# Linear attention, gated feed-forward and four attention experts on one core: scores of head pairs without the later quarter, block-diagonal values, k loaded by halves, and the experts' mask over 128 rows

## Chip, cores and metric

One core of one Trainium2 chip runs the whole program. The metric is the device time of one execution in microseconds; less is better. The kernel before has a median of 767.92 us over three runs (767.56 to 768.51).

## What is computed

Four batches (B = 4) of 768 tokens pass through three stages, all in float32.

1. Linear attention of 8 heads with head size 48. With a complex decay a, brought to a magnitude of at most 0.999, a state of 48 x 48 per head follows `S_t = a_t * S_(t-1) + k_t v_t^T`, and `y_t = q_t . Re(S_t)`.
2. Feed-forward: `h = relu(x @ w_in)` of width 1024, a convolution over 3 tokens, a sigmoid of it as a gate, and `(h * gate) @ w_out`, which has width 384.
3. Four experts of one attention head each (size 64) with a causal mask. Scores are `q k^T / 8`, softmax over keys, `@ v @ wo`; each token adds the two experts with the highest gate logits, weighted.

## The kernel before, in words

**Chunks.** The recurrence is worked out in 6 chunks of 128 tokens (NC, CH). The cumulative products of the decays are taken from the middle of a chunk outwards, so q and k are scaled once and inside a chunk the outputs are a masked product: scores = k^T q (L1427), multiplied by a 0/1 mask (L1086) and used as the moving operand of a product with v. A token of a chunk lies in one of two halves of 64 (HALF), so that partitions 0 to 63 of a chunk's tokens are its first half and 64 to 127 its second. What came before the chunk enters through a state `st` of 96 rows (real and imaginary part of 48).

**One chunk on TensorE** (`main` of the tensor block): `scores(c+1)`, 8 products of 96 rows x 128 keys x 128 queries into two PSUM banks; `transpose_k(c+1)`, 8 transposes (L1414); `rotate(c)` (L1451); `outputs(c, 0)`; `gain(c+1)`, 8 products of 128 tokens x 96 x 48 columns (L1439); `outputs(c, 1)`; `outputs(c, 2)`. An output block packs four products with 32 stationary columns side by side into the array (L1478 with v as stationary operand, L1476 with the state). Blocks 0 and 1 take the first or last 32 columns of v of four heads each, block 2 the remaining 16 of each head in pairs that are summed, over columns padded with zeros. Every f32 product that is no transpose is two instructions in the trace.

**One chunk on the other engines.** VectorE masks the scores in two instructions, one per four heads (`mask`, L1086), and makes the state of the next chunk (L1104, L1119, L1122, L1124) and the low part of x (`x_low`, L1095). ScalarE copies the transposed k (`copy_k`, L639) and the outputs (`copy_x`, L647). In batches 1 and 2 it does parts of the next batch's decays between chunks: after `copy_x` of chunk 3 it loads a table, takes square roots (L596), loads another table, takes a logarithm and an exponential (L600, L605), and only then comes to `copy_x` of chunk 4.

**Queues.** All transfers are issued by SyncE (SP), in program order. q and k are stored scaled to DRAM, and `load_heads(b, c)` fetches a chunk of them by head into one of three slots (L496), as four transfers of 48 rows: q and k, real and imaginary. A slot is free when the outputs of the chunk three before are ready. In batch 0 the stores of units 1 and 2 (`store_first_chunk`, `store_unit`, L483, L473) and the loads of the next batch's decays (`load_a`, L439) stand between the loads of the chunks.

**Experts.** Twelve steps t per batch, each with two query tiles (sides 0 and 1) that together see 7 x 128 keys. `expert_scores(t)` makes the scores of side 1, adds the mask to them (`later`, L1591), then makes those of side 0 (512 keys at most per product, so two products where it has 768 or 640 keys) and masks these. An expert's q and k lie in 64 rows of the array, and the experts of the two sides always lie in different halves. The mask is a product of two bf16 operands of 64 rows, in two instructions. The order of the work is written out by hand: in step t, TensorE makes the scores of t + 2, transposes the probabilities of t (L1617), and makes a product with v every second time (L1633) and the output projection (L1641).

The functions that the change touches:

## Time and profile before

| | |
|---|---|
| median of the runs | 767.92 us (767.56 to 768.51) |
| the profiled execution | 768.12 us |
| its span in the profile | 766.2 us |
| TensorE busy with products | 671.0 us, 88% of the span |
| TensorE busy with weight loads (beside the products) | 511.4 us, 67% |
| VectorE busy | 614.7 us, 80% |
| ScalarE busy | 409.2 us, 53% |
| chain that ended last, by engine | TensorE 45%, VectorE 36%, ScalarE 8%, DMA 5% |

The profile lists busy time per engine. A product's duration contains its way through the array, so products overlap in it, and what a product costs in a stream is read from the distance of the starts or from the chain of waits. That chain is followed back from the last instruction: each piece was released by the end of the one before it. A batch takes 168 us in the steady state: linear attention about 41 us, the feed-forward stage 54 us and 23 us with the projections, the experts 50 us. "PE" is TensorE, "PEld" its weight loads, "DVE" VectorE, "ACT" ScalarE, "SPq" the queue of SyncE.

### The profile page before, as it was taken

Reading aid. Unit: us, or ns where it says so; the run is one execution under the profiler, and the core shown is the slowest. Engines: PE = TensorE matmul, PEld = TensorE weight load, DVE = VectorE, ACT = ScalarE, POOL = GpSimd, SP = SyncE. Lnnn points to the kernel's source line nnn. Section 1 sums busy time; section 2 is a strip of 40 time slices with the busy share of each in tenths; the row PEclk is TensorE's granted clock in tenths of the full one; section 3 lists DMA queues with packets and bytes.
Section 4 is the critical chain, followed back from the end, with each engine's and each line's share of the span. In section 5 each row is a group of like instructions: output and inputs, shape, how many; then the busy total and the mean of one; then the engine's idle time right before and its main releaser. Section 6 shows DMA issues by size and latency. Waiting matters only on the chain.

```text
span 766.2 us, 13280 instructions
## 1 busy us (share of the span) xinstructions
PE 671.0 (88%) x5274; PEld 511.4 (67%) x5274; DVE 614.7 (80%) x1165; ACT 409.2 (53%) x747; POOL 0.2 (0%) x4
## 2 busy tenths in 40 slices
PE   0006868799999999999999999999999999999998
PEld 0003657676656778876656788876667788998765
DVE  3999876899889878899888878899888675773563
ACT  6304237633757854533757756434766434664565
POOL 0000000000000000000000000000000000000000
PEclk9999898999999999999999999999999999999999
DMA  8604684310018473500028653300027440000001
GB/s 345 254 0 119 175 234 138 123 42 0 1 41 227 148 197 75 178 29 1 0 63 248 175 158 111 139 1 0 1 86 224 126 121 8 1 1 1 1 22 42
DMA packets 93629, 73.85 MB, mean 96 GB/s; under 512 B 8704, under 2 KB 85760, under 8 KB 92928
## 3 DMA queue, kind: packets, MB, share of 16 engines
q1 hardware_dynamic: 93568, 73.01, 31.4%
q8 instruction: 42, 0.69, 0.4%
q14 instruction: 19, 0.16, 0.1%
HBM read 49.34 MB, written 23.65 MB: 95 GB/s over the span
## 4 chain that ended last, share of the span: by engine, by line
PE 45%; DVE 36%; ACT 8%; DMA 5%; issue 3%; SPq 2%; DVEq 0%; ACTq 0%
DVE cv L1131 7%; PE wide L1582 5%; PE wide L1563 5%; PE bank L1633 4%; PE bank L1641 4%; PE wide L1617 4%; PE wide L1427 4%; DVE m L949 3%; DVE heads L1136 3%; PE wide L1439 3%; DMA heads_dram<-araw 3%; DVE m L948 2%; DVE nmax L1195 2%; PE wide L1558 2%; DVE W L961 2%
## 5 line engine op out<-in xcount | busy, mean ns | idle before, releaser
L1492 PE MATMUL wide<-x_hi_lo,win_hi 128*128 128x384 f32 x384 | 108.9, 353 | 7.9 <-DVE x_hi_lo L1095 6.6
L1492 PEld LDWEIGHTS wide<-x_hi_lo,win_hi 128*128 128x128 f32 x384 | 70.7, 190 | 12.5 <-issue 8.5
L1513 PE MATMUL wide<-heads,wout 128*128 128x384 f32 x200 | 70.7, 496 | 4.1 <-DVE heads L1136 4.0
L1195 DVE TENSOR_REDUCE nmax<-wide 128x1 f32<-128x768 f32 (+2 forms) x96 | 55.3, 618 | 23.3 <-PE wide L1591 23.1
L1131 DVE SCALAR_TENSOR_TENSOR cv<-h,wconv,cv 128x768 f32<-128x768 f32 x64 | 64.9, 1014 | 8.2 <-ACT cv L679 6.7
L1582 PE MATMUL wide<-attn 64*128 64x512 f32 (+3 forms) x256 | 65.0, 482 | 2.3 <-ACT attn L703 2.3
L727 ACT ACTIVATE xs<-wide 128x896 f32<-128x896 f32 x48 | 44.1, 919 | 41.6 <-PE wide L1617 41.6
L1492 PE MATMUL wide<-x_hi_lo,win_lo 128*128 128x384 f32 x192 | 65.1, 339 | 0.0
L1427 PE MATMUL wide<-heads 96*128 96x128 f32 x384 | 52.0, 292 | 10.3 <-DMA heads<-heads_dram 10.3
L684 ACT ACTIVATE cv<-cv 128x768 f32<-128x768 f32 x32 | 27.1, 845 | 58.3 <-DVE cv L1131 58.1
L1427 PEld LDWEIGHTS wide<-heads 96*128 96x128 f32 x384 | 48.3, 203 | 14.8 <-DMA heads<-heads_dram 11.0
L1401 PE MATMUL wide<-attn,ident 128*128 128x512 f32 x4 | 3.1, 860 | 62.2 <-ACT m L621 62.2
L1513 PEld LDWEIGHTS wide<-heads,wout 128*128 128x128 f32 x200 | 36.2, 189 | 30.9 <-DVE heads L1136 11.0
L657 ACT ACTIVATE h<-wide 128x384 f32<-128x384 f32 x64 | 29.0, 489 | 50.7 <-DVE heads L1136 39.2
L1633 PE MATMUL bank<-xs,attn 128*64 128x128 f32 x672 | 46.4, 279 | 0.2 <-ACT xs L727 0.2
L1086 DVE TENSOR_TENSOR attn<-wide,cmask 128x512 f32<-128x512 f32 x48 | 31.3, 682 | 17.2 <-PE wide L1427 17.2
L1633 PEld LDWEIGHTS bank<-xs,attn 128*64 128x64 f32 x672 | 35.8, 136 | 13.5 <-ACT xs L727 8.1
L1401 PEld LDWEIGHTS wide<-attn,ident 128*128 128x128 f32 x4 | 1.0, 289 | 63.0 <-issue 63.0
L1582 PEld LDWEIGHTS wide<-attn 64*128 64x128 f32 x256 | 25.5, 184 | 24.1 <-issue 9.9
L718 ACT ACTIVATE cv<-wide,nmax 128x768 f32<-128x768 f32 (+2 forms) x48 | 37.9, 790 | 1.0 <-DVE nmax L1195 0.5
L1617 PE MATMUL wide<-ident,cv 128*128 128x128 f32 x240 | 36.6, 283 | 2.0 <-DVE cv L1210 2.0
L1492 PEld LDWEIGHTS wide<-x_hi_lo,win_lo 128*128 128x128 f32 x192 | 36.6, 190 | 2.0
(205 smaller groups left out, 1512.6 us busy)
## 6 DMA issues: line engine op xcount, KB each, us to landing
heads<-heads_dram SPq DMA_DIRECT2D x96, 192.0 KB, 3.5
araw<-a_in SPq DMA_DIRECT2D x12, 768.0 KB, 6.2
araw<-qk_in SPq DMA_DIRECT2D x12, 768.0 KB, 4.8
heads_dram<-m SPq DMA_DIRECT2D x18, 384.0 KB, 3.4
heads_dram<-araw SPq DMA_DIRECT2D x18, 384.0 KB, 4.0
v<-v_in SPq DMA_DIRECT2D x4, 1536.0 KB, 6.6
out_dram<-h SPq DMA_DIRECT2D x24, 192.0 KB, 2.5
heads_dram<-m SPq DMA_DIRECT2D x12, 192.0 KB, 3.5
```

What stands on the lines that cost most here:

```text
L718: nc.scalar.activation(prob[side][:, t % 2, 0:n], slot_scores(t, side), ACT.Exp, bias=nmax[:, t, side:side + 1], accum_out=zsum[:, t, side ...
L727: nc.scalar.activation(probT[:, t % PROBT, :], wide[2][:, 0:KEYS], ACT.Copy).then_inc(s_pc, 1)
L1086: TT(sc[:, c % 2, 4 * quad:4 * quad + 4, :], low[2 + quad].rearrange("p (h t) -> p h t", h=4), cmask[:].unsqueeze(1).broadcast_to([P, 4, P ...
L1131: STT(cb, hb[:, tap:tap + S], wconv[:, mt, tap:tap + 1], cb, ALU.mult, ALU.add).then_inc(s_c, 1)
L1195: dve.tensor_reduce(nmax[:, t, side:side + 1], slot_scores(t, side), AXX, ALU.max, negate=True).then_inc(s_nm, 1)
L1427: last = MM(low[2 + quad][:, hh * P:(hh + 1) * P], k_of(c, hd), q_of(c, hd), start=True, stop=True)
L1492: last = MM(low[u % 2][:, 0:NT], w[:, k, mt * P:(mt + 1) * P], xs[:, k, n * NT:(n + 1) * NT], start=(k == 0 and part == 0), stop=(k == KT ...
L1513: last = MM(mlp_bank[u][:, 0:NT], wout[:, mt, k * P:(k + 1) * P], hgate(mt)[:, n * NT:(n + 1) * NT], start=(mt == 0), stop=(mt == MT - 1))
L1563: last = MM(bank_u[:, 0:NT], w[:, k, i * P:(i + 1) * P], xT[:, k, n * NT:(n + 1) * NT], start=(k == 0), stop=(k == KT - 1))
L1582: MM(slot_scores(t, side)[:, lo:hi], qT[rows, e // 2, i * P:(i + 1) * P], kT[rows, e // 2, lo:hi], start=True, stop=hi != keys(t, side))
L1617: last = nc.tensor.transpose(dst[:, j * P:(j + 1) * P], prob[side][:, t % 2, j * P:(j + 1) * P], ident[:])
L1633: last = MM(out_bank[side][rows, o:o + P], vx[:, j, e * HD:(e + 1) * HD], probT[:, (t + r) % PROBT, span(t, side)][:, j * P:(j + 1) * P], ...
```

## The change

- **Scores.** A pair of heads gets three squares of a half chunk each instead of two full 128 x 128 squares: in one PSUM strip of 192 columns the rows 0 to 63 belong to the first head of the pair and 64 to 127 to the second. Keys of the first half meet all 128 queries, keys of the second half only the 64 later queries. There are 16 products with 64 stationary columns where 8 had 128.
- **Mask.** VectorE multiplies the two outer planes of each strip in one instruction (512 columns, mask in bf16); ScalarE copies the middle plane (`copy_scores`, 256 columns), which needs no mask. TensorE's next scores and outputs wait for this copy (semaphore s_sf), and the copy waits for the mask. In ScalarE's order `copy_scores(b, 0)` comes first in a batch, and `copy_scores(b, c+1)` after `copy_k(b, c+1)`.
- **Values.** v is stored block-diagonally: for each pair and half, 128 rows (two heads x 64 tokens) by 96 columns, 4608 columns per partition in place of 3072. `gain` has 8 products of 96 columns where 8 had 48. Output blocks 0 and 1 take 64 stationary columns of a pair and half, with 128 or 64 query columns; block 2 takes the last 32 columns of each pair. The state's products in blocks 0 and 1 become 6 per block in place of 4, in block 2 4 in place of 8. The weights w_in are reordered to match.
- **k by halves.** `load_heads` issues six transfers in place of four: k comes in two halves of 64 tokens.
- **Experts' mask.** `later` is one product over all 128 rows in place of two over 64, and for side 1 it now comes after the first product of side 0. The wait for it before the second product of side 0 stays.
- Small things: lf, gt, the gates' small buffers and the third staging buffer of w_in lie in other buffers; the mask constants are fewer; `keep_busy` has 384 columns in place of 512; the mask is cast to bf16 once, before the first `mask`.

The core of the diff:

```diff
@@ -81,6 +81,8 @@
 SHORT = PAIRS * P
 KEYS = (NC + 1) * P
 PROBT = 4
+PAIR = 3 * HALF
+HEAD_PARTS = 16 * 6
 HOLD = 3
...
@@ -103,11 +105,10 @@
         ident = sb("ident", [P, P])
-        negated = sb("negated", [P, P])
-        cmask = sb("cmask", [P, P])
+        cmask = sb("cmask", [P, P], BF16)
         rot = sb("rot", [2 * D, 2 * D])
         tie = sb("tie", [P, E * E])
...
@@ -288,6 +289,7 @@
         s_te = sem("k_tokens_copied")
         s_s = sem("scores_ready")
         s_se = sem("scores_masked")
+        s_sf = sem("scores_copied")
...
@@ -348,8 +350,13 @@
         def groups(part):
             return part.rearrange("p (n i g) -> p n i g", i=GROUP, g=GROUP)
-        def k_of(c, hd):
-            return qk_slot[:, c % SLOTS_A, 1, hd, :]
+        def k_half(c, half):
+            return qk_slot[:, c % SLOTS_A, 1, half * H // 2:(half + 1) * H // 2, :].rearrange("d h t -> d (h t)")
+        def k_of(c, hd, half):
+            return k_half(c, half)[:, hd * HALF:(hd + 1) * HALF]
...
@@ -359,6 +366,23 @@
             return t[:, hd, 0:D]
+        def pair_values(c, p, half):
+            return v[:, c, p, half, :]
+        def pair_scores(p):
+            return wide[1][:, p * 2 * P:p * 2 * P + PAIR]
+        def pair_planes(t, size):
+            return t.rearrange("p (n x) -> p n x", x=size)[:, :, 0:PAIR].rearrange("p n (r x) -> p n r x", x=HALF)
...
@@ -491,10 +515,14 @@
                     sp.wait_ge(s_sto[c // UNIT_CHUNKS], 64 * (b + 1))
                 if c >= SLOTS_A:
                     sp.wait_ge(s_y, NC * b + c - SLOTS_A + 1)
-                for x in range(2):
-                    for part in range(2):
-                        sp.dma_start(qk_slot[part * D:(part + 1) * D, c % SLOTS_A, x, :, :],
-                                     qk_dram[x, part, c].rearrange("(h d) t -> d h t", d=D)).then_inc(s_hd[c % SLOTS_A], 16)
+                for part in range(2):
+                    rows = slice(part * D, (part + 1) * D)
+                    sp.dma_start(qk_slot[rows, c % SLOTS_A, 0, :, :],
+                                 qk_dram[0, part, c].rearrange("(h d) t -> d h t", d=D)).then_inc(s_hd[c % SLOTS_A], 16)
+                    for half in range(2):
+                        sp.dma_start(k_half(c, half)[rows].rearrange("d (h t) -> d h t", h=H),
+                                     qk_dram[1, part, c, :, half * HALF:(half + 1) * HALF]
...
@@ -639,6 +667,15 @@
                     nc.scalar.activation(ktok[:, c % 2, part * DM:(part + 1) * DM], low[part][:, 0:DM],
                                          ACT.Copy).then_inc(s_te, 1)
+            def copy_scores(b, c):
+                act.wait_ge(s_se, NC * b + c + 1)
+                if c >= 2:
+                    act.wait_ge(s_y, NC * b + c - 1)
+                nc.scalar.activation(pair_planes(sc[:, c % 2].rearrange("p h t -> p (h t)"), PAIR)[:, :, 1, :],
+                                     pair_planes(wide[1][:], 2 * P)[:, :, 1, :], ACT.Copy).then_inc(s_sf, 1)
             def copy_x(b, c):
...
@@ -742,9 +779,13 @@
             def main(b):
                 more = b + 1 < B
+                if b:
+                    copy_scores(b, 0)
                 for c in range(NC):
                     if c + 1 < GAINS:
                         copy_k(b, c + 1)
+                    if c + 1 < NC:
+                        copy_scores(b, c + 1)
                     if b and more and c < UNITS - 1:
...
@@ -888,6 +929,7 @@
             w_squares(0, 2)
             w_ln(0, 2)
             w_guess(0, 2)
+            copy_scores(0, 0)
             for b in range(B):
...
@@ -1078,14 +1120,15 @@
                     TT(araw[:, x, cols], araw[:, x, cols], w_re[:, cols], ALU.mult).then_inc(done, 1)
             def mask(b, c):
-                for quad in range(2):
-                    n = 2 * (NC * b + c) + quad
-                    dve.wait_ge(s_s, n + 1)
-                    if c >= 2:
-                        dve.wait_ge(s_y, NC * b + c - 1)
-                    TT(sc[:, c % 2, 4 * quad:4 * quad + 4, :],
-                       low[2 + quad].rearrange("p (h t) -> p h t", h=4),
-                       cmask[:].unsqueeze(1).broadcast_to([P, 4, P]), ALU.mult).then_inc(s_se, 1)
+                dve.wait_ge(s_s, NC * b + c + 1)
+                if c >= 2:
+                    dve.wait_ge(s_y, NC * b + c - 1)
+                TT(pair_planes(sc[:, c % 2].rearrange("p h t -> p (h t)"), PAIR)[:, :, 0::2, :],
+                   pair_planes(wide[1][:], 2 * P)[:, :, 0::2, :],
+                   cmask[:].rearrange("p (r x) -> p r x", x=HALF).unsqueeze(1).broadcast_to([P, H // 2, 2, HALF]),
+                   ALU.mult).then_inc(s_se, 1)
...
@@ -1375,6 +1417,9 @@
                 products_by_chunk(u, 0)
                 if u == 1:
                     w_sumsq(0, UNITS - 1)
+                    dve.wait_ge(s_const, 64)
+                    dve.tensor_copy(cmask[:], staged[:, 0:P]).then_inc(s_cast, 1)
+                    dve.wait_ge(s_cast, 3)
                     mask(0, 0)
...
@@ -1391,7 +1436,7 @@
                 for _ in range(n):
-                    MM(b6[:], ident[:], mask_parts, start=True, stop=True)
+                    MM(b6[:, 0:3 * P], ident[:], staged, start=True, stop=True)
...
@@ -1407,26 +1452,30 @@
                 n = 2 * (GAINS * b + c) + part
                 if part == 0:
-                    pe.wait_ge(s_hd[c % SLOTS_A], 64 * (2 * b + c // SLOTS_A + 1))
+                    pe.wait_ge(s_hd[c % SLOTS_A], HEAD_PARTS * (2 * b + c // SLOTS_A + 1))
                 if c:
                     pe.wait_ge(s_te, n - 1)
-                for hh in range(4):
-                    last = nc.tensor.transpose(low[part][:, hh * 2 * D:(hh + 1) * 2 * D], k_of(c, 4 * part + hh),
-                                               ident[0:2 * D, 0:2 * D])
+                for i in range(4):
+                    p, half = 2 * part + i // 2, i % 2
+                    last = nc.tensor.transpose(low[part][:, i * 2 * D:(i + 1) * 2 * D],
+                                               k_half(c, half)[:, p * P:(p + 1) * P], ident[0:2 * D, 0:2 * D])
                 last.then_inc(s_t, 1)
             def scores(b, c):
-                for quad in range(2):
-                    n = 2 * (NC * b + c) + quad
-                    if c and quad == 0:
-                        pe.wait_ge(s_hd[c % SLOTS_A], 64 * (2 * b + c // SLOTS_A + 1))
-                    if c:
-                        pe.wait_ge(s_se, n - 1)
-                    for hh in range(4):
-                        hd = 4 * quad + hh
-                        last = MM(low[2 + quad][:, hh * P:(hh + 1) * P], k_of(c, hd), q_of(c, hd),
-                                  start=True, stop=True)
-                    last.then_inc(s_s, 1)
+                if c:
+                    pe.wait_ge(s_hd[c % SLOTS_A], HEAD_PARTS * (2 * b + c // SLOTS_A + 1))
+                    pe.wait_ge(s_sf, NC * b + c)
+                for p in range(H // 2):
+                    for half in range(2):
+                        for r in range(2):
+                            hd = 2 * p + r
+                            cols = slice(P * half, P * half + (HALF if half else P))
+                            last = MM(pair_scores(p)[r * HALF:(r + 1) * HALF, cols],
+                                      k_of(c, hd, half), q_of(c, hd)[:, half * HALF:],
+                                      start=True, stop=True)
+                last.then_inc(s_s, 1)
             def gain(b, c):
@@ -1435,9 +1484,11 @@
                 else:
                     pe.wait_ge(s_u, GAINS * b + c)
                 pe.wait_ge(s_te, 2 * (GAINS * b + c) + 2)
-                for hd in range(H):
-                    last = MM(b5[0:2 * D, hd * D:(hd + 1) * D], ktok[:, c % 2, hd * 2 * D:(hd + 1) * 2 * D],
-                              values(v[:, c], hd), start=True, stop=True)
+                for p in range(H // 2):
+                    for half in range(2):
+                        i = 2 * p + half
+                        last = MM(b5[0:2 * D, p * 2 * D:(p + 1) * 2 * D], ktok[:, c % 2, i * 2 * D:(i + 1) * 2 * D],
+                                  pair_values(c, p, half), start=half == 0, stop=half == 1)
                 last.then_inc(s_z, 1)
             def rotate(b, c):
@@ -1462,20 +1513,36 @@
                         pe.wait_ge(s_fe[0], PAIRS * b + 1)
                     if c:
                         pe.wait_ge(s_st, GAINS * b + c)
-                if block < 2:
-                    pe.wait_ge(s_se, 2 * n + block + 1)
-                take = remaining if block == 2 else leading
-                heads_of = [[4 * block + g for g in range(4)]] if block < 2 else [[2 * g + r for g in range(4)] for r in range(2)]
+                if block == 0:
+                    pe.wait_ge(s_sf, n + 1)
                 o = y_bank[c % 2][:, block * P:(block + 1) * P]
-                for part in range(2 if c else 1):
-                    for r, some in enumerate(heads_of):
-                        first_one, last_one = part == r == 0, (part == 1 or c == 0) and r == len(heads_of) - 1
-                        for g, hd in enumerate(some):
-                            dst = o[g * LEAD:(g + 1) * LEAD, :]
-                            if part:
-                                last = MM(dst, take(st[:, c % 2], hd), q_of(c, hd), start=first_one, stop=last_one)
-                            else:
-                                last = MM(dst, take(v[:, c], hd), sc[:, c % 2, hd, :], start=first_one, stop=last_one)
+                for g in range(2 if block < 2 else 4):
+                    p = 2 * block + g if block < 2 else g
+                    rows, cols = ((slice(2 * LEAD * g, 2 * LEAD * (g + 1)), slice(0, 2 * LEAD)) if block < 2 else
+                                  (slice(LEAD * g, LEAD * (g + 1)), slice(2 * LEAD, 3 * LEAD)))
+                    first_half, second_half = (pair_values(c, p, half)[:, cols] for half in range(2))
+                    some = sc[:, c % 2, p, :]
+                    if c:
+                        MM(o[rows, :], first_half, some[:, 0:P], start=True, stop=False)
+                    else:
+                        MM(o[rows, 0:HALF], first_half, some[:, 0:HALF], start=True, stop=True)
+                        MM(o[rows, HALF:P], first_half, some[:, HALF:P], start=True, stop=False)
+                    last = MM(o[rows, HALF:P], second_half, some[:, P:PAIR], start=False, stop=c == 0)
+                if c:
+                    state = st[:, c % 2]
+                    if block < 2:
+                        pairs = (2 * block, 2 * block + 1)
+                        parts = ([(2 * g, leading(state, 2 * p), 2 * p, True) for g, p in enumerate(pairs)]
+                                 + [(2 * g + 1, remaining(state, 2 * p + r), 2 * p + r, r == 1)
+                                    for r in range(2) for g, p in enumerate(pairs)])
+                    else:
+                        parts = [(p, leading(state, 2 * p + 1), 2 * p + 1, True) for p in range(H // 2)]
+                    for g, weights, hd, ends in parts:
+                        last = MM(o[g * LEAD:(g + 1) * LEAD, :], weights, q_of(c, hd), start=False, stop=ends)
                 if block == KT - 1:
                     last.then_inc(s_y, 1)
...
@@ -1585,17 +1652,14 @@
                 def later(side):
-                    i, e = query_tile(t, side), expert(t, side)
-                    rows = slice(HD * (e % 2), HD * (e % 2) + HD)
-                    for r in range(2):
-                        last = MM(slot_scores(t, side)[:, i * P:(i + 1) * P], mask_h[rows, r * P:(r + 1) * P],
-                                  mask_h[rows, (2 + r) * P:(3 + r) * P], start=False, stop=r == 1)
-                    return last
+                    i = query_tile(t, side)
+                    return MM(slot_scores(t, side)[:, i * P:(i + 1) * P], mask_h[:, 0:P], mask_h[:, P:2 * P],
+                              start=False, stop=True)
                 n = keys(t, 0)
                 products(1, 0, keys(t, 1))
+                products(0, 0, 512)
                 later(1).then_inc(s_sh, 1)
-                products(0, 0, 512)
                 if n > 512:
                     pe.wait_ge(s_sh, SLOTS * b + t + 1)
```

## Rows read from the trace of the kernel before

**Rows 1.** Busy time by stage: us, then PE, PEld, DVE, ACT, POOL busy, clock, DMA share, GB/s.
```profile
433.00:474.00 41.00, 40.71 (x613) 34.33 (x611) 33.32 (x58) 23.76 (x38) 0.00 (x0) 1.00 0.49 131
614.60:621.41 6.81, 6.81 (x108) 5.79 (x107) 5.02 (x9) 2.39 (x5) 0.00 (x0) 1.00 0.44 116
```

**Rows 2.** Chain of waits, one chunk of batch 3: start us, us, what.
```profile
614.60 1.98 PE wide L1427 x16
616.58 0.66 PE wide L1414 x8
617.24 0.65 PE bank L1451 x2
617.89 0.36 PE bank L1478 x8
618.25 0.22 PE bank L1476 x8
618.47 1.49 PE wide L1439 x16
...
620.53 0.44 PE bank L1478 x16
620.97 0.44 PE bank L1476 x16
```

**Rows 3.** The same chain in batch 1: scores at its start, a wait in its second chunk.
```profile
265.24 1.81 PE wide L1427 x16
...
280.11 5.85 DMA heads<-heads_dram
```

**Rows 4.** Timeline of the SP queue in batch 0: start us, us, operation, transfers.
```profile
77.91 1.86 SPq L496 DMA_DIRECT2D heads<-heads_dram  x4
...
80.87 1.32 SPq L483 DMA_DIRECT2D heads_dram<-araw  x2
...
116.57 2.10 SPq L496 DMA_DIRECT2D heads<-heads_dram  x4
118.78 0.55 SPq L439 DMA_DIRECT2D araw<-a_in  x1
```

**Rows 5.** Timeline of ScalarE in batches 0 and 2; in brackets its idle time.
```profile
125.17 1.49 ACT L591 ACTIVATE m<-araw 128x1536 f32<-128x1536 f32 x1 [0.38 <-DMA araw<-a_in]
...
441.24 0.49 ACT L741 ACTIVATE h<-bank 128x384 f32<-128x384 f32 x1 [0.80 <-PE bank L1641]
...
468.33 1.28 ACT L596 ACT_TABLE_LOAD   x1
...
473.50 0.86 ACT L647 ACTIVATE x_hi_lo<-wide 128x192 fp32r<-128x192 f32 x2
```

**Rows 6.** Timeline of TensorE in batch 2: start of the second chunk's scores, end of the stage.
```profile
441.04 1.95 PE L1427 MATMUL wide<-heads 96*128 96x128 f32 x16
...
472.17 0.43 PE L1478 MATMUL bank<-attn,v 128*32 128x128 f32 x8 [0.29 <-issue]
...
476.41 0.41 PE L1492 MATMUL wide<-x_hi_lo,win_hi 128*128 128x384 f32 x1 [0.51 <-DVE x_hi_lo L1095]
```

**Rows 7.** Timeline of TensorE, one step of the experts in batch 3.
```profile
730.79 0.71 PE L1582 MATMUL wide<-attn 64*128 64x256 f32 x3
731.33 0.22 PE L1591 MATMUL wide<-mask_h 64*128 64x128 bf16 x1
...
731.77 0.38 PE L1582 MATMUL wide<-attn 64*128 64x128 f32 x2
...
732.19 0.76 PE L1617 MATMUL wide<-ident,cv 128*128 128x128 f32 x5
```

**Rows 8.** Groups by form: copies and masks; count, busy us, mean ns, idle before.
```profile
L697 ACT ACTIVATE attn<-wide 128x256 f32<-128x256 f32 x16 | 6.1, 384 | 5.1 <-PE wide L1558 3.7 <-PE wide L1554 1.3
L1086 DVE TENSOR_TENSOR attn<-wide,cmask 128x512 f32<-128x512 f32 x48 | 31.3, 682 | 17.2 <-PE wide L1427 17.2
```

**Rows 9.** The page's transfers: KB each, median us from issue to landing.
```profile
heads<-heads_dram SPq DMA_DIRECT2D x96, 192.0 KB, 3.5
```

86 lines of the change are left out of this document (41 added, 45 removed).

## The prediction

> **What bounds the kernel now.** I read the stages first, then the chain of waits, then the timelines at the places where the change puts something new. In the linear attention of a steady batch the stage table has TensorE busy for 40.71 of 41 us, VectorE for 33.32, ScalarE for 23.76; in one chunk of 6.81 us TensorE has no gap at all [rows 1]. The chain says the same: all ten pieces of a chunk are products (the two left out repeat the 0.36 and 0.22), and they add up to those 6.81 us [rows 2]. So in this stage a microsecond counts if it is TensorE's; the vector engine's 5.02 us per chunk lie beside it. Three places differ. In batch 0 the chain runs through SP's queue and its transfers, up to the load of decays at 118.78 that releases ScalarE at 125.17 [rows 4, 5]. In batch 1 it waits once 5.85 us for a chunk's heads [rows 3]. At the end of batches 1 and 2 it runs through ScalarE, which after chunk 3's copy does 5.2 us of the next batch's decays before it copies chunk 4 [rows 5]. In the experts' later steps it is TensorE again.
>
> **What a product costs here.** A chunk's scores take 16 instructions in 1.81 us where no changeover of the array precedes them, 0.111 to 0.113 us each with 128 stationary and 128 moving columns [rows 3]; after packed products they take 1.98, so a changeover costs about 0.15. The gain has 96 stationary and only 48 moving columns, and its 16 still take 1.49 us, less the changeover 0.084 each: 0.87 ns per stationary column, so there the weights set the pace, and scores are at the same 0.87 ns per column [rows 2]. Packed products with 32 stationary and 128 moving columns come every 0.0275 us, a quarter of 0.11 [rows 2]. I take the rule that an instruction costs the larger of 0.85 ns per stationary column and 0.85 ns per moving column over the number of products side by side.
>
> **The change, TensorE's part.** Scores: 32 instructions of 64 stationary columns, 0.054 each by that rule, 1.73 us against 1.78: -0.05. The quarter that is left out shortens only the moving side; if weights of neighbouring tiles load at the same time, the price is (16 x 0.054 + 16 x 0.027) = 1.3 us, -0.5. Nearest row is the gain, weight-bound, so I take -0.05. The transposes after the scores now follow a packed product: one changeover, +0.12 (0 to 0.2, from the 0.17 between the two score rows). Output blocks 0 and 1: the values' 8 instructions have 64 stationary columns, 0.43 against 0.22, +0.21 each (+0.1 if moving columns count); the state's products with 32 columns follow those with 64, +0.12 each if this is a changeover (0 to 0.17), and are 12 in place of 8, +0.11 each (+0.2 if the two that share 32 columns of the array queue up). Block 2: the values stay at 16 instructions, 0.44 by the weights; the state's halve, -0.22. The gain keeps 96 stationary columns and gets 96 moving ones: 0 by the rule; the transposes with 128 stationary and 96 moving columns run at 0.66/8 = 0.083, which also fits [rows 2]; +0.1 at worst. Sum: -0.05 + 0.12 + 0.42 + 0.24 + 0.22 - 0.22 = +0.7 us per chunk (-0.3 to +1.3). Chunk 0 has no state, but its first product is split in two, so that blocks have 12, 12 and 24 instructions in place of 8, 8 and 16: about +0.9 with scores and changeover.
>
> At the changeover between tile widths the rows show 1.98 against 1.81 us for the same scores [rows 2, 3], but no row has 64 columns followed by 32. The Trainium skill, TensorEngine Tiling (Array Packing), section Key Properties, says that changing the tiling mode, not merely the tile, drains the engine; by it both widths in a block cost as in my sum. Without it the sum would be 0.24 less per chunk. The same section says that different tiles can load weights and multiply in parallel, which speaks for the lower price of the scores; that is a rival below.
>
> On the path lie, in batches 1 to 3, three chunks 0 (2.7 us), nine full chunks (two in batch 1, three in batch 2, four in batch 3; 6.3 us) and the outputs of batch 3's last chunk (0.6): **+9.6**. Batch 0's chunks lie under its transfers, and the chunks 4 and 5 of batches 1 and 2 under ScalarE's chain, counted next.
>
> **The new waits on ScalarE.** (a) Start of a batch: scores of chunk 1 now wait for the copy of chunk 0's middle plane, which stands behind the last output copy of the batch before. That copy runs from 441.24 to 441.73 [rows 5]; 256 columns take 0.384 [rows 8]; with the hand-over the scores start at about 442.2 in place of 441.04 [rows 6]: +1.2, three times, **+3.6**. The mask is done long before, and behind the waiting TensorE stands only its own order. (b) End of batches 1 and 2: the copy for chunk 5 stands behind the decays of the next batch, that is from 473.5 [rows 5]. Chunk 5's outputs started at 472.17 [rows 6]; now they start at 473.5 + 0.45 + 0.05 = 474.0 plus what the chunks before are late. They take 2.6 us, copy and low part 0.9 each, so the first product that needs chunk 5 starts at 478.6 in place of 476.41 [rows 6]: 2.2, and the table load behind the copy adds 0.2: +2.4, twice, **+4.8**. (c) In the other chunks the copy has a whole chunk's time; hidden by TensorE's 6.8 us, and 0.4 us per chunk if that cover were gone.
>
> **SP's queue.** An issue takes 1.86 / 4 to 2.10 / 4 us, 0.5 [rows 4]. Two more per chunk: in batch 0 the loads of chunks 0 and 1 push the four stores behind them from the end of the load at 79.8 to 81.9; two of these had waited for VectorE until 80.87 and now start at 82.9, +2.0. Chunks 2 to 5 add 1.0 each, all ahead of the load at 118.78, and ScalarE had only 0.38 us idle there [rows 4, 5]. **+6.0**. ScalarE must also have copied chunk 5's plane before these squares; that is about as late, 0 to +2, taken in the range. In batch 1 the wait of 5.85 us [rows 3] begins 1.0 later and its transfers have half the row length for k: **+1.2**. Elsewhere a chunk's load takes 0.35 + 5 x 0.5 + 3.5 to 5.85 us (median landing [rows 9], and this row), 6.4 to 8.7, against a period of 7.5; at the median it fits.
>
> **The experts.** In a step with 640 keys TensorE needs 1.40 us from the first scores to the transposes [rows 7]. Side 1's scores and side 0's run beside each other in different halves of rows, so side 0 sets the time: about 0.1 + 0.85 + 0.21 + mask. Now the mask over 128 rows waits until both have drained (0.1), passes through (0.22 [rows 7]), and only its end releases the next product (weights and hand-over 0.13), then the array changes over twice (0.2) and one mask instruction instead of two is saved (0.06): 1.8 us, +0.4, the same with 768 keys; without a second product (512 keys) about 0. Eight steps of batch 3 are bound by TensorE: 3.2. In batches 0 to 2 the first two are (0.8), four more are bound by VectorE and TensorE alike (half, 0.8), the others hidden: 4.8. **+8.0** (0 to 13).
>
> **Costed at nothing:** 24 masks fewer on VectorE, 0.68 us each [rows 8], hidden under TensorE, and worth 0.65 once before the first chunk, against the cast of the mask; v's larger rows and the moved small buffers lie in front of loads that the feed-forward stage covers; 384 columns in `keep_busy` fill a wait for a transfer. If the cover of v's load were gone it would cost its extra 0.8 MB, some 3 us per batch at the rate of its own loads.
>
> Sum: 9.6 + 3.6 + 4.8 + 6.0 + 1.2 + 8.0 = 33.2 on the profiled 768.12 us: 801.3. The median of the runs is 0.2 lower, so **801 us**.
>
> **Rivals.**
> - *The tiles load side by side and changing width is free.* Then scores fall by 0.5, values' blocks rise by 0.2 together and block 2 falls by 0.1: with the one changeover -0.3 per chunk in place of +0.7, chunk 0 at 0. For it: 32-column products at 0.0275 would also come out so. Against it: the gain. Nothing outside the loop changes: 33.2 - 12.8 = 20.4, **788**. Chance 0.27.
> - *The heads' transfers become the bound.* If they land in 5.85 us as in batch 1 [rows 3], a chunk takes 8.7 us in place of 7.5, three chunks in each of three batches: +10, **811**. Against it: the median landing of 3.5 [rows 9]. Chance 0.12.
> - *VectorE was the real pace of the loop.* Freed of one mask per chunk, 0.64 x 18 = 11.5 us less, **757**, if none of the additions shows. It decides once a chunk's masks, not its products, end last; at 5.02 of 6.81 us busy, and with no VectorE piece in the chain [rows 1, 2], little speaks for it. Chance 0.06.
> - *Gains and waits cancel*, 768, which needs the weights' rule and the queue's both wrong. Chance 0.03.
> - My forecast: 0.52.
>
> **Numbers.** The range reaches from below the first rival (experts' step at nothing: 780) to above the second with batch 0's extra wait (817). Within 0.2%, 1.5 us, is what a measurement of this kernel can't tell from no change. Faster 0.06, same 0.03, slower 0.91.
>
> **What would show it.** The score group: 768 instructions with 64 stationary columns at 0.05 us apart, or at 0.04. The chunk period in batch 3: 7.5 us, against 6.5 for the first rival. A ScalarE wait of 1.2 us before the scores of chunk 1, and chunk 5's outputs released by ScalarE's copy in batches 1 and 2. The start of the products with w_in in batch 0 some 6 us later. An idle 0.3 to 0.5 us behind the mask product in each expert step with 640 or 768 keys. If the period is below 6.8 or the time below 780, the price per stationary column was wrong.

## The result and the profile after

The changed kernel has a median of 803.01 us over four runs (802.2 to 805.07), the kernel before in the same series 768.08. The ratio is 1.0454, with a 95% interval of 1.0431 to 1.0476: slower, 2.0 us above the forecast of 801.0 and inside the range. The profiled execution has a span of 800.9 us, 34.7 more than before; the comparisons by stage below are made with spans. One execution of experiment 4 and one of experiment 5 lie far above the others of their kernel; their medians are those of the other three, and both are named below.

The page of the changed kernel: span, busy time per engine, chain by engine, the group of the row maxima (count, busy us, mean ns, idle before and its releaser), and the heads' transfers.

```profile
span 800.9 us, 14033 instructions
PE 701.2 (88%) x5626; PEld 511.3 (64%) x5626; DVE 602.2 (75%) x1142; ACT 416.2 (52%) x771; POOL 0.2 (0%) x4
PE 51%; DVE 28%; ACT 8%; DMA 6%; issue 4%; SPq 3%; DVEq 0%; ACTq 0%
L1238 DVE TENSOR_REDUCE nmax<-wide 128x1 f32<-128x768 f32 (+2 forms) x96 | 55.3, 618 | 33.6 <-PE wide L1656 33.5
heads<-heads_dram SPq DMA_DIRECT2D x48, 192.0 KB, 3.0
heads<-heads_dram SPq DMA_DIRECT2D x96, 96.0 KB, 3.2
```

TensorE is busy 30 us longer and its share of the chain rises from 45% to 51%, while VectorE's busy time falls by 12.5 us and its share of the chain from 36% to 28%. The time still rose: the loop had no VectorE piece in its chain before [rows 2], so the masks that VectorE was spared could give little back there. Transfers of k with half the rows' length and half the bytes land in 3.2 us, against 3.5 for whole ones before [rows 9]: they did not become the bound.

**One chunk in batch 3**, in the chain of waits (start us, us, what). It answers to [rows 2].

```profile
644.24 1.49 PE wide L1475 x32
645.73 0.81 PE wide L1460 x8
646.54 0.65 PE bank L1502 x2
647.18 0.38 PE bank L1528 x4
647.56 0.11 PE bank L1532 x4
647.67 0.57 PE bank L1545 x12
648.25 1.53 PE wide L1490 x16
649.78 0.38 PE bank L1528 x4
650.15 0.11 PE bank L1532 x4
650.27 0.36 PE bank L1545 x8
...
651.43 1.09 PE wide L1475 x21
```

The period is 651.43 - 644.24 = 7.19 us against 6.81. Piece by piece: scores 1.49 against 1.98 (-0.49), transposes 0.81 against 0.66 (+0.15), values of block 0 0.49 against 0.36 (+0.13), its state 0.57 against 0.22 (+0.35), gain +0.04, blocks 1 and 2 together 1.65 against 1.45 (+0.20). The sum is +0.38; TensorE still has no gap.

**The three stages of each batch.** From the timelines of TensorE I took the first score, the first product with w_in, the first projection, and the next batch's first score. (Of batch 0 the first two stages stand together.) The feed-forward stage has the same length in both within 0.1 us. The column "more" is taken before rounding. Each row comes from one profile, and moves a little from profile to profile: experiments 5, 6, 7 and 9 below change nothing in batch 0 up to the projections (7 only an order inside the chunk), and there it takes 200.7, 200.4, 203.8 and 202.6 us.

| stage | before | after | more | forecast |
|---|---|---|---|---|
| batch 0 up to the projections | 197.1 | 202.1 | +5.0 | +6.0 |
| attention, batch 1 | 41.3 | 45.8 | +4.5 | +7.1 |
| attention, batch 2 | 40.6 | 46.7 | +6.1 | +6.6 |
| attention, batch 3 | 40.5 | 44.2 | +3.6 | +5.5 |
| projections and experts, batch 0 | 68.0 | 74.4 | +6.4 | +1.6 |
| batch 1 | 68.0 | 72.1 | +4.1 | +1.6 |
| batch 2 | 68.0 | 70.4 | +2.4 | +1.6 |
| batch 3, to the end | 70.7 | 73.6 | +2.9 | +3.2 |

The rows add to 35.0, with the rounding of the feed-forward stages 34.7. The forecast total was near, its parts were not: attention cost 5 us less than it said, the experts 8 more, nearly all in batches 0 and 1. There the chain of the changed kernel has pieces that the kernel before does not have; this is batch 0's end:

```profile
256.95 4.03 DMA heads_dram<-araw
261.00 0.33 SPq L520
...
263.94 6.10 DMA araw<-a_in
...
271.45 0.91 ACT xs L764
```

VectorE's products for the next batch end later, their store lands later, SP then issues six loads of heads (2.9 us), and behind them the second third of the decays of batch 2 at 263.94, and ScalarE's squares wait for that. In the kernel before, the same load was issued 10.1 us sooner, of which batch 0's late start explains 5.0:

```profile
253.84 0.55 SPq L439 DMA_DIRECT2D araw<-a_in  x1
```

The transposed probabilities (L764) stand behind the squares. ScalarE's timeline has the wait in brackets:

```profile
270.06 1.48 ACT L619 ACTIVATE m<-araw 128x1536 f32<-128x1536 f32 x1 [2.28 <-DMA araw<-a_in]
```

### The profile page after: what moved, and what is told of

Its sections match the earlier page's. It is cut to its first block, busy times and chain, and to the rows that moved or that the text cites. A ratio compares the mean times of both kernels' runs of the same rounds, so it can differ in the third digit from the quotient of the medians.

```text
span 800.9 us, 14033 instructions
## 1 busy us (share of the span) xinstructions
PE 701.2 (88%) x5626; PEld 511.3 (64%) x5626; DVE 602.2 (75%) x1142; ACT 416.2 (52%) x771; POOL 0.2 (0%) x4
## 4 chain that ended last, share of the span: by engine, by line
PE 51%; DVE 28%; ACT 8%; DMA 6%; issue 4%; SPq 3%; DVEq 0%; ACTq 0%
PE wide L1649 8%; DVE cv L1174 7%; PE wide L1630 4%; PE bank L1697 4%; PE wide L1681 4%; DMA heads_dram<-araw 3%; PE wide L1475 3%; DVE m L991 3%; PE wide L1490 3%; PE bank L1705 3%; DVE heads L1179 3%; PE wide L1559 2%; DVE m L990 2%; DMA araw<-a_in 2%; PE wide L1625 2%
## 5 line engine op out<-in xcount | busy, mean ns | idle before, releaser
L1238 DVE TENSOR_REDUCE nmax<-wide 128x1 f32<-128x768 f32 (+2 forms) x96 | 55.3, 618 | 33.6 <-PE wide L1656 33.5
L1649 PE MATMUL wide<-attn 64*128 64x512 f32 (+3 forms) x256 | 73.1, 495 | 4.2 <-ACT attn L740 2.3
L1580 PE MATMUL wide<-heads,wout 128*128 128x384 f32 x200 | 70.7, 496 | 4.2 <-DVE heads L1179 4.2
L764 ACT ACTIVATE xs<-wide 128x896 f32<-128x896 f32 x48 | 44.0, 917 | 49.5 <-PE wide L1681 49.5
L1475 PE MATMUL wide<-heads 96*64 96x128 f32 (+1 forms) x768 | 39.9, 260 | 10.9 <-DMA heads<-heads_dram 8.0
L1475 PEld LDWEIGHTS wide<-heads 96*64 96x64 f32 x768 | 36.7, 144 | 16.5 <-DMA heads<-heads_dram 8.5
L1681 PE MATMUL wide<-ident,cv 128*128 128x128 f32 x240 | 34.9, 276 | 4.0 <-ACT xs L764 4.0
L1580 PE MATMUL bank<-heads,wout 128*128 128x384 f32 x100 | 36.3, 486 | 0.0
```

What stands on the lines that cost most here:

```text
L764: nc.scalar.activation(probT[:, t % PROBT, :], wide[2][:, 0:KEYS], ACT.Copy).then_inc(s_pc, 1)
L1238: dve.tensor_reduce(nmax[:, t, side:side + 1], slot_scores(t, side), AXX, ALU.max, negate=True).then_inc(s_nm, 1)
L1475: last = MM(pair_scores(p)[r * HALF:(r + 1) * HALF, cols], k_of(c, hd, half), q_of(c, hd)[:, half * HALF:], start=True, stop=True)
L1580: last = MM(mlp_bank[u][:, 0:NT], wout[:, mt, k * P:(k + 1) * P], hgate(mt)[:, n * NT:(n + 1) * NT], start=(mt == 0), stop=(mt == MT - 1))
L1649: MM(slot_scores(t, side)[:, lo:hi], qT[rows, e // 2, i * P:(i + 1) * P], kT[rows, e // 2, lo:hi], start=True, stop=hi != keys(t, side))
L1681: last = nc.tensor.transpose(dst[:, j * P:(j + 1) * P], prob[side][:, t % 2, j * P:(j + 1) * P], ident[:])
```

## The experiments

Twelve kernels ran. "Before" was run beside each set of four: median 769.27 us beside experiments 1 to 4, 768.66 beside 5 to 8 and 768.95 beside 9 to 12. No kernel leaves computation out.

**1. k by halves alone**, on the kernel before (wait counts adapted):

```diff
-                for x in range(2):
-                    for part in range(2):
-                        sp.dma_start(qk_slot[... x, :, :], qk_dram[x, part, c] ...)
+                for part in range(2):
+                    sp.dma_start(qk_slot[rows, c % SLOTS_A, 0, :, :], qk_dram[0, part, c] ...)
+                    for half in range(2):
+                        sp.dma_start(qk_slot[rows, c % SLOTS_A, 1, :, cols], qk_dram[1, part, c, :, cols] ...)
```

> The kernel before, with each chunk's k loaded by halves of its tokens (six transfers of heads per chunk in place of four, rows of 256 bytes for k), everything else as before. Theory: SP's queue is on the path. In batch 0 ten of the added issues at 0.5 us stand ahead of the load of decays that ScalarE waits for, +5 us; in batch 1 the wait for chunk 3's heads grows by 1.2; and in the experts of batches 0 and 1 the decays' loads, which stand behind the heads' in the queue, may now be late for ScalarE, +0 to 4. So 774 to 778, and the start of the w_in products of batch 0 some 5 us later. Rival: the queue is late only together with TensorE's own delay; then 768 to 770.

Measured: 774.34 us (seven executions, 771.0 to 782.1), ratio 1.0082 (1.0039 to 1.0125). The size is right, the place is right only in part. Batch 0 up to the projections stays at 197.1: the load of decays that [rows 4] has at 118.78 is issued at 119.45, because SP's added issues filled time in which it had waited for stores. The cost came at the experts' end in batches 0 and 1 (70.2 and 72.8 in place of 68.0, 7.0 us in the profile, where 0 to 4 had been expected) and 1.0 in the attention of batches 1 and 2. The chain at the end of batch 1 has the pieces that were shown above for the changed kernel:

```profile
420.56 4.85 DMA heads_dram<-araw
...
429.05 5.98 DMA araw<-a_in
```

**2. The experts' mask alone**, on the kernel before: one product over 128 rows, for side 1 after the first product of side 0 (the mask's constants and the width of `keep_busy` follow).

```diff
-                    for r in range(2):
-                        last = MM(..., mask_h[rows, r * P:(r + 1) * P], mask_h[rows, (2 + r) * P:(3 + r) * P], ...)
+                    return MM(..., mask_h[:, 0:P], mask_h[:, P:2 * P], start=False, stop=True)
...
-                later(1).then_inc(s_sh, 1)
                 products(0, 0, 512)
+                later(1).then_inc(s_sh, 1)
```

> The kernel before with only the experts' mask of the change: one product over 128 rows, and for side 1 behind the first product of side 0. Theory: in steps with 640 and 768 keys the second product of side 0 waits for the mask to pass through the array; about +0.3 to 0.4 us in the steps that TensorE bounds, in all +6 to +10, 774 to 778, with a step of 640 keys in batch 3 at 1.8 us from scores to transposes in place of 1.40. Rival: the saved mask instructions pay for the wait; 766 to 769.

Measured: 779.5 us, ratio 1.0135 (1.0107 to 1.0162), 1.5 above the expected 774 to 778. The experts take 70.3, 71.5, 70.3 in batches 0 to 2 and 73.6 in batch 3: +2.3 to 2.9 where only the mask acts, and in batch 1 1.2 more by the load of decays (7.35 us in the chain).

**3. The same mask at its old place**, ahead of side 0's product:

> As the last one, but with the mask of side 1 in its old place, before the products of side 0. If the wait for the mask was the cost, this takes it away (it is covered by side 0's first product) and the time comes back to 766 to 770. If the cost is that a product over all 128 rows can't run beside the other side's, side 1 and side 0 now run one after the other: +0.3 to 0.7 us per step, in all 48 steps, so slower than the late order, 780 to 790.

Measured: 797.82 us, ratio 1.0375 (1.0336 to 1.0414), worse than any bound that I had set. The experts take 75.5 in batches 0 to 2, +7.5 each, and 78.9 to the end in batch 3, +8.2. TensorE's timeline of a step with 640 keys:

```profile
761.10 0.70 PE L1582 MATMUL wide<-attn 64*128 64x256 f32 x2
761.73 0.23 PE L1589 MATMUL wide<-mask_h 128*128 128x128 bf16 x1
761.89 1.34 PE L1582 MATMUL wide<-attn 64*128 64x512 f32 x4
...
763.24 0.72 PE L1614 MATMUL wide<-ident,cv 128*128 128x128 f32 x5
```

From the first score to the transposes it takes 2.14 us (before: 1.40 [rows 7]). The mask over 128 rows starts behind side 1's scores, and side 0's only start behind the mask, 0.79 us after side 1's: the two sides no longer run beside each other in their halves of the rows. At its late place the same mask cost 18 us less (experiment 2).

**4. The middle plane copied by VectorE**, on the changed kernel (ScalarE's calls of `copy_scores` taken out):

```diff
+                dve.tensor_copy(pair_planes(sc[...], PAIR)[:, :, 1, :],
+                                pair_planes(wide[1][:], 2 * P)[:, :, 1, :]).then_inc(s_sf, 1)
```

> The changed kernel with the middle plane of the scores copied by VectorE right behind its mask instruction; ScalarE has no part in it. Theory: the waits on ScalarE go: 0.9 us at the start of batches 1 to 3, and at the end of batches 1 and 2 about 3 us each with the slow clock behind it; in all -9 to -11, so 792 to 794, although VectorE has 0.4 us more per chunk. Rival: VectorE's added copy is on the path itself, or what is behind ScalarE's (its own decays) is as late; 799 to 803.

Measured: 790.0 us (three executions, 789.6 to 791.4), ratio 1.0277 (1.0244 to 1.0311), 13 us less than the changed kernel and below the 792 to 794 expected. A fourth execution, the profiled one, took 2368 us (see the end), so this kernel has no trace from which its stages can be read; experiments 8 and 10 contain the same edit.

**5. The first third of the decays ahead of the heads**, on the changed kernel:

```diff
+                    if b + 2 < B:
+                        load_a(b + 2, 0)
                     sp.wait_ge(s_p, len(PROJECTIONS) * (b + 1))
                     load_heads(b + 1, 0)
                     load_heads(b + 1, 1)
-                    if b + 2 < B:
-                        load_a(b + 2, 0)
```

> The changed kernel, but the load of the decays for the batch after next (its first third) is issued ahead of the twelve loads of heads of chunks 0 and 1, in batches 0 and 1. Theory: part of the time lost in the experts of batches 0 and 1 is not the mask but the queue: this load, 6.1 and 5.9 us from issue to landing in the chain of the changed kernel, releases ScalarE's squares, and it stood 4 us of issues late; put first it is off the chain, and 4 to 7 us come back: 796 to 799 us. Rival (the mask's wait alone makes the experts longer, the load only happens to end last): 802 to 804, unchanged. The profile should show ScalarE's squares in these stages no longer released by the load of decays.

Measured: 798.8 us (three executions, 797.8 to 800.8; a fourth took 934.4 at a mean granted clock of 0.76), ratio 1.0397 (1.0376 to 1.0419): -4.2. The total fell into the expected range, but only in part for its reason, since I had moved the load before the one that waits. In batch 0 the squares start at 267.20 in place of 270.06 and are off the chain (experts 71.4 in place of 74.4). They are still held in batch 1, where the chain still has the second third, at 438.40 for 5.93 us; everything ahead of it was 4 us sooner than in the changed kernel. Experiment 9 moves the right load.

**6. Transposes in the wait for the mask**, on the changed kernel:

```diff
                 later(1).then_inc(s_sh, 1)
+                if then:
+                    then()
                 if n > 512:
...
-                        expert_scores(b, t + 2)
-                    transpose_probs(b, t)
+                        expert_scores(b, t + 2, lambda: transpose_probs(b, t))
```

> The changed kernel, but in each expert step the transposes of the probabilities of two steps before are issued between the first mask product and the second product of side 0, where TensorE waits for the mask. Theory: the 0.3 to 0.5 us between the mask and the next product is a wait, so other work put there hides it, 12 steps with more than 512 keys in batch 3 and as many in the others, of which about half are bound by TensorE: -2 to -5 us, 798 to 801. Rival: the loss is the drain and changeover around the mask and the loss of products side by side, which the transposes don't cover, and the row maximum waits 0.8 us longer for its scores: 803 to 808.

Measured: 817.04 us, ratio 1.0632 (1.0614 to 1.0649). The expected gain did not come, the rival did, and at 14 us nearly three times as dear as its upper end. VectorE's row maxima now wait longer for their scores (51.2 us in all, 33.6 in the changed kernel), and TensorE in turn for the probabilities, which it did not before. The group of the row maxima:

```profile
L1238 DVE TENSOR_REDUCE nmax<-wide 128x1 f32<-128x768 f32 (+2 forms) x96 | 55.4, 618 | 51.2 <-PE wide L1656 51.2
```

And a row of TensorE's timeline, in brackets its wait:

```profile
776.32 0.74 PE L1683 MATMUL wide<-ident,cv 128*128 128x128 f32 x5 [0.67 <-DVE cv L1253]
```

The edit puts the transposes ahead of side 0's last scores and mask in every step, so also in those with 512 keys, which had no wait to cover. The rows fit a loop of scores, maximum, scaling and transposes with so little slack that covering 0.3 us on TensorE costs more on the way round. Whether the wait itself could be covered by work outside this loop was not tried.

**7. One more change of tile width per chunk**, on the changed kernel: in block 1 the state's products go ahead of the values'.

```diff
+                late = block == 1 and c > 0
...
+                if late:
+                    from_state()
+                    last = from_values()
```

> The changed kernel, but in output block 1 the state's products (32 columns) go ahead of the values' (64 columns). The work is the same; TensorE changes its tile width once more per chunk: 128, 32, 64, 32 in place of 128, 64, 32, 32. Theory (a change of width costs 0.12 to 0.15 us whichever widths they are): the chunk grows by 0.12 to 0.15, 12 to 13 chunks on the path: +1.5 to +2, 804.5 to 805. Rival (only 128 against packed tiles costs, between 64 and 32 it is free): 803 and the chunk of batch 3 stays at 7.19 us.

Measured: 803.04 us, ratio 1.0442 (1.0415 to 1.0468), no difference that the runs can show; the step is too small for them. The trace shows it. A chunk in the same place of batch 3:

```profile
643.20 1.49 PE wide L1475 x32
...
648.73 0.57 PE bank L1549 x12
649.31 0.38 PE bank L1531 x4
649.68 0.12 PE bank L1535 x4
...
650.51 1.49 PE wide L1475 x32
```

The period is 7.31 against 7.19: +0.12 for one change more between 32 and 64 columns. By the rival the period would have stayed.

**8. Experiments 4 and 5 together:**

> The changed kernel with both edits: the middle plane copied by VectorE, and the load of decays ahead of the loads of heads. Theory: ScalarE's waits (12 us by the run before) and the queue (4 to 7) are different places, so they add: 784 to 787. In batch 0 the squares after chunk 5 are then released by the load of decays again, at about 127 in place of 130 us, because in the changed kernel it was the copy behind the masks of chunk 5 that held them, not SP's queue, whose two more loads per chunk delayed the load of decays by only 1.9 us. Rival (the two overlap, the queue's part is hidden once ScalarE is free): 789 to 791.

Measured: 793.04 us (788.77 to 797.12), ratio 1.0318 (1.0267 to 1.0368). They don't add: the rival, and even its 789 to 791 is met by only two of the four executions. In batch 0 the squares start at 125.91 and the projections at 198.5 (changed kernel 202.1), about as expected, though what releases the squares is ScalarE's copy of the outputs and not the load. Attention in batches 2 and 3 takes 43.1 and 43.2. But batch 1's attention takes 49.9: the heads of chunk 3 stand in the chain for 5.54 us, and behind that wait TensorE works much of a chunk at the lower clock (see the end).

**9. The second third of the decays ahead of the heads of chunk 2**, on the changed kernel:

```diff
                 if more:
-                    load_heads(b + 1, 2)
                     if b + 2 < B:
                         load_a(b + 2, 1)
+                    load_heads(b + 1, 2)
```

> The changed kernel, but in batches 0 and 1 the load of the second third of the decays is issued ahead of the six loads of heads of chunk 2, not behind them; both wait for the same store. (The run before had moved the first third, which is the one issued before it.) Theory: this is the load that ends the chain in these two stages, issued 2.94 us after the store has landed; in front, ScalarE's squares start 2.9 us sooner in each, less what the next wait takes (ScalarE's own copy at 268.6 us in batch 0): -4 to -6 us, 797 to 799. Rival (the store of the products before it is what is late, and the transfer shares its time with the heads': the gain is lost in a slower landing): 801 to 803.

Measured: 796.83 us, ratio 1.0361 (1.0333 to 1.0389): -6.2. The experts take 70.4 in batch 0 and 70.4 in batch 1, as in batch 2 (74.4 and 72.1 in the changed kernel). ScalarE's squares run without a wait, at 268.11:

```profile
267.74 0.50 ACT L778 ACTIVATE h<-bank 128x384 f32<-128x384 f32 x1
268.11 1.50 ACT L619 ACTIVATE m<-araw 128x1536 f32<-128x1536 f32 x1
```

This settles the experts: +2.4 a batch is the mask's price, and the 5.7 us on top in batches 0 and 1 are this load. (The size of that wait depends on when the batch began: in experiment 7, with the same queue, batch 0 began its projections 1.7 later and the experts took 72.3 and 71.7, 3.2 on top.) The attention of batch 1 became 1.3 longer (47.1), since it now waits for the heads of chunk 3 (5.33 us in the chain), which the delay had hidden.

**10. Experiments 4 and 9 together:**

> The same with the middle plane copied by VectorE. Theory: 790.7 less 4 to 6: 785 to 787, about 17 us above the kernel before; what is left is then the mask, the products and the queue's part in the loop. Rival, after the run that moved the first third (it gave 789 in half of its executions and 796 in the others): nothing is gained, because batch 1's first chunks then wait for their heads, 5.5 us in the chain: 790 to 796.

Measured: 791.18 us, ratio 1.0291 (1.0255 to 1.0326): the rival. With the queue in order, VectorE's copy is worth 5.6 us and not 13; without ScalarE's waits, the queue's order is worth nothing that these runs can show (791.2 against 790.0). Attention takes 43.1 in batches 2 and 3, but 45.1 in batch 1, with this in its chain:

```profile
277.19 6.31 DMA heads_dram<-araw
...
288.78 5.36 DMA heads<-heads_dram
```

Whatever starts batch 1 sooner meets the same stores and loads of its decays and heads.

**11. Experiment 2 with the second third moved**, on the kernel before:

> The kernel before with only the experts' mask of the change (128 rows, its late place), and the load of the second third of the decays ahead of the loads of heads of chunk 2. Theory: of the 10.4 us that this mask cost alone, some 4 to 6 are not TensorE's but this load, which stood in the chain for 7.35 us in batch 1; then 774 to 776, and the rest (5 to 7 us) is the wait for the mask, by batch as in batches 2 and 3. Rival: all is TensorE's, 779.

Measured: 778.7 us (five executions, 777.7 to 783.1), ratio 1.0122 (1.0096 to 1.0149): by the time, the rival, but its reason, that all is TensorE's, doesn't hold in this profile. The experts of batch 1 fall from 71.5 to 70.3, so the load is off the chain there; but batch 1's attention takes 45.3 in place of 42.1, again with a wait for its heads (6.65 us), and the scores after it take 2.90 us, at a mean granted clock of 0.67. The profiled execution is the slowest of the five, 4.4 us above their median, so how much of this wait the others have is not shown.

**12. Experiments 1 and 2 together**, on the kernel before:

> The kernel before with two parts of the change, k loaded by halves (six transfers a chunk) and the mask over 128 rows. Theory: alone they cost 6.3 and 10.4 us and partly in the same place, the load of decays behind the loads of heads in batches 0 and 1, where one wait takes in the other or lengthens it: 783 to 786 for the sum, so that ScalarE's waits (12) and the products (6) make up the rest of the 34.7. Rival (they share one wait and only the longer counts): 780 to 782.

Measured: 785.59 us, ratio 1.0211 (1.018 to 1.0243). The two add (5.1 + 10.2 = 15.3 over the first set's 769.27, here 16.6). The experts of batches 0 and 1 take 73.9 each, close to the changed kernel's 74.4 and 72.1. The 17 us left to 803 are then ScalarE's copy and the products, with v's rows and the moved buffers, which no run took alone.

## Why the prediction was right, and where not

*Right: the direction, the bound of the loop, ScalarE's waits.* TensorE's products stayed the bound of the loop, and both waits on ScalarE that the forecast named are in the trace. Two terms of SP's queue are not (below).

*The products' price per stationary column was wrong.* It priced 32 instructions with 64 stationary columns at 0.054 each and took -0.05 for the scores; they came to 1.49 us, -0.49, of which the first rival had the rule. What fits all packed groups is the moving side of each tile by itself: scores have 4 pairs x (128 + 64) columns x 2 instructions per tile. At 0.86 ns per column, from four packed instructions of 128 columns in 0.11 us [rows 2], that is 1.32 us, with a changeover 1.45; the state's 12 instructions put four of 128 columns on one tile, 4 x 0.11 + 0.13 = 0.57, as measured. So the forecast's larger-of rule may stand for each tile by itself; what was wrong was to add up the weight loads of neighbouring tiles, as if they took turns. No run changed the products alone. The gain, which had spoken against this, uses the array as one tile. The Trainium skill, TensorEngine Tiling (Array Packing), section Key Properties, says that different tiles can load weights and multiply in parallel; the 1.49 us agree.

*The changeover was right.* +0.15 at the transposes (forecast 0.12), and experiment 7 shows 0.12 between 64 and 32 columns. So the first rival was right in its first half and wrong in its second. The same section of the Trainium skill says that a change of tiling mode drains the engine; the 0.12 agree, as far as a cost can. The blocks' sums came out, +0.48 in block 0 (forecast 0.44) and +0.20 in blocks 1 and 2 (0.22), but by luck: in block 0 the values cost 0.13 more and not 0.21, the state 0.35 and not 0.23, because two of its products queue up on one tile. Chunk 0 takes 6.68 against 5.82 from scores to scores, +0.9 as forecast. (In the first rival's own sum, its terms give 12.2 less and not 12.8; that makes 789 of its 788.) With +0.38 in place of +0.7 nine chunks cost 3.4 and not 6.3 us.

*ScalarE's wait at a batch's start was sized about right*, 0.94 us where the forecast had 1.2. TensorE's last output product ends, then:

```profile
636.58 0.49 ACT h L778
637.07 0.28 ACT attn L676
...
637.49 1.56 PE wide L1475 x32
```

*ScalarE's wait at the end of batches 1 and 2 is there too.* In batch 2 ScalarE's timeline has the decays and then the copy:

```profile
495.12 0.84 ACT L633 ACTIVATE m<-m 128x768 f32<-128x768 f32 x1
495.86 0.36 ACT L676 ACTIVATE attn<-wide 128x256 f32<-128x256 f32 x1
```

Chunk 5's outputs start at 496.37, released by this copy after TensorE had stood idle for 1.60 us (0.29 before [rows 6]), and the first products after that are worked at a granted clock below full. TensorE's row, and then the windows (length, busy times, then the clock):

```profile
496.37 0.45 PE L1528 MATMUL bank<-attn,v 128*64 128x128 f32 x4 [1.60 <-ACT attn L676]
...
496.00:500.02 4.02, 3.65 (x65) 2.94 (x65) 0.91 (x2) 0.99 (x3) 0.00 (x0) 0.76 0.00 0
500.02:507.30 7.28, 7.28 (x38) 7.28 (x39) 4.45 (x10) 4.60 (x8) 0.00 (x0) 0.90 0.84 319
```

In experiment 9, with the same wait of 1.60 us but the clock at 1.00 after it, batch 2's attention takes 45.8, 1.6 more than batch 3's; here, with the lower clock, it takes 46.7, 2.5 more, against the forecast 2.4. The kernel before has the clock at 1.00 at this place. So in batch 2 the term was met by a smaller wait and a clock that the forecast had not counted; in batch 1, at full clock, it was about 1.6. VectorE's copy takes all of this away (43.1 in both batches).

*SP's queue in batch 0: the size is right, the cause is wrong.* The forecast moved every issue by what stood ahead of it, +6.0; the load of decays was issued at 120.69 in place of 118.78, +1.9, and experiment 1, with the same queue, lost nothing there. What cost the time is two other things. From chunk 4's scores to chunk 5's, TensorE works at about half the clock (from 114.68 to 127.00: 0.54; in the kernel before it was back at 1.00 from 120 on). Behind it comes the term that the forecast had put "about as late, 0 to +2, taken in the range": ScalarE's copy of chunk 5's plane. The chain:

```profile
129.61 0.38 ACT attn L676
129.99 1.37 ACT m L619
```

The squares start at 129.99 instead of 125.17 [rows 5]. Experiments 8 and 10, without ScalarE's copy, share this out. In experiment 10 the clock is as low as here (0.50 from 120 to 125), and the squares start at 128.01:

```profile
128.01 1.28 ACT m L619
```

In experiment 8 it comes back sooner (0.71 from 120 to 125), and they start at 125.91. So the copy is about 2 of the 4.8 us, and the longer stretch at the lower clock 2.8. That low clock isn't the change's alone: experiment 11 leaves the chunks as they were and has 0.50 there too.

*The queue elsewhere: the step that failed.* "Elsewhere ... at the median it fits" looked at the loop alone. At the experts' end six issues stand between the landing of a store and the load that ScalarE needs, and the mask and batch 0's late start make that store later; this cost 5.7 us (experiment 9). The +1.2 for batch 1's wait for heads didn't come: the delay ahead of it hid the wait, and it returns, as 5.3 to 6.7 us in the chain, in experiments 8 to 11 as soon as the delay is taken away.

*The experts: the working of a step was right.* TensorE's timeline of a step with 640 keys, which answers to [rows 7]:

```profile
764.87 1.13 PE L1649 MATMUL wide<-attn 64*128 64x256 f32 x4
765.94 0.23 PE L1656 MATMUL wide<-mask_h 128*128 128x128 bf16 x1
766.22 0.49 PE L1649 MATMUL wide<-attn 64*128 64x128 f32 x2
766.64 0.23 PE L1656 MATMUL wide<-mask_h 128*128 128x128 bf16 x1
766.71 0.71 PE L1681 MATMUL wide<-ident,cv 128*128 128x128 f32 x5
```

From the first score to the transposes 1.84 us, forecast 1.8; batch 3 lost 2.9, forecast 3.2. In batches 0 to 2 the forecast took half of four steps as VectorE's (1.6), and they cost nearly as much as in batch 3 (2.4).

So the total came out near by luck, because errors cancelled: the score products' price (3 us too much), the wait for heads (1.2 too much), and the load of decays behind the heads (5.7 us not seen), besides 2.4 of the experts' steps. And batch 0's +5.0 met its +6.0 by another cause. Of the rivals, the second (transfers as the bound) and the third (VectorE as the pace) are out: transfers land in 3.2 us, and VectorE lost 12.5 us of work while the time rose.

No kernel here beats the one before. The best of the changed ones (790.0 and 791.2) still carry the mask (about 10 us), the products of the chunks (2.6 us in batches 2 and 3, by 43.1 against 40.5) and batch 1's wait for its heads. The scores' own saving, 0.49 us a chunk, was not tried alone. What is left open is how the 13 us of experiment 4 are shared out, since it has no usable trace of its own. Experiments 9 and 10 differ by 5.6 in their medians and by 7.5 in their profiles: 1.8 in batch 0, 2.0 in batch 1, 2.7 in batch 2, 1.0 in batch 3.

## What to carry to other kernels

Price packed products by the tile, each with its moving columns, and add one changeover for each change of width; what fewer columns save in one group is quickly eaten by more products and changeovers in the next. A term that gives a stage back its slack must be followed round to the next batch: here more issues in the queue, or a later store behind a mask on TensorE, each alone turned a load that had been on time into a wait on ScalarE (experiments 1 and 2). And where two waits gate the same start, removing one is worth little and removing both may uncover a third, so measure them together before adding up.

## What was not expected of the hardware

- After a short wait TensorE's granted clock is at the lower of its two levels (1.2 GHz) in some executions and not in others. In experiment 8's profile it waited 2.10 us for heads and worked the next chunk in 11.8 us instead of 7.2, its scores at 0.50:

```profile
293.59:296.40 2.81, 2.81 (x33) 2.69 (x33) 0.00 (x0) 0.08 (x1) 0.00 (x0) 0.50 0.90 196
```

  In experiment 10 it waited 1.86 us at the same place and kept the full clock. In one profile of the changed kernel itself it waited 1.60 us at the end of batch 1 and of batch 2, and only behind the second was the clock lower. Experiment 8's four executions took 788.8 and 790.1 us at a mean clock of 0.987 and 0.989, and 796.0 and 797.1 at 0.976. A spread like that hides a few us of gain or loss.
- One execution of experiment 4 took 2368 us. The profile shows the granted clock at 1.00 throughout, VectorE's instructions at their usual duration (row maxima 619 ns) and TensorE busy for 99.8% of the stretch below; its products took 2 to 3 times their duration in every group. Nothing in the kernel that I know of explains it, and the three other executions agree within 0.3%.

```profile
1000.00:2000.00 1000.00, 997.91 (x2597) 509.32 (x2596) 243.11 (x469) 173.06 (x330) 0.00 (x0) 1.00 0.10 29
L1556 PE MATMUL wide<-x_hi_lo,win_hi 128*128 128x384 f32 x384 | 311.1, 931 | 0.0
```
